# Zero fills spread over eight load steps instead of four, and row stores two steps later, in a kernel of attention and two expert layers

## What is computed

```python
# attention: B, H, S, D = 4, 8, 768, 48
for t in range(S):
    kt, vt, rt = (k[:, :, t], v[:, :, t], r[:, :, t])
    cur = np.einsum('bhd,bhe->bhde', u[None] * kt, vt)
    y[:, :, t] = np.einsum('bhd,bhde->bhe', rt, state + cur)
    state = w[None, :, :, None] * state + np.einsum('bhd,bhe->bhde', kt, vt)

# experts: N, D, E, F = 3072, 384, 8, 1024
e_idx = np.argmax(x @ w_gate, axis=1)
for e in range(E):
    mask = e_idx == e
    h = np.maximum(x[mask] @ w1[e], 0.0)
    out[mask] = gate_w[mask, None] * eom[mask, e, None] * (h @ w2[e])

# feed-forward: 3072 x 384, width 1536
g = x @ w_gate
val = x @ w_val
out = (silu(g) * val) @ w_out
```

## Time and profile before

| what | us |
|---|---|
| median of 3 runs (932.32 to 932.51) | 932.42 |
| the profiled execution, whole | 924.97 |
| its span, first to last instruction | 922.8 |
| PE busy in the span | 852.6 (92%) |
| DVE busy | 362.8 (39%) |
| POOL busy | 276.7 (30%) |
| ACT busy | 249.6 (27%) |
| attention stage, start to the first load of sorted rows | 184.2 |

### The profile page before, as it was taken

One profiled execution on the slowest core, in us unless ns is written; L12 is line 12 of the kernel. 1 busy time (PEld: TensorE's weight loads), 2 busy tenths in 40 slices (PEclk: granted clock), 3 DMA queues, 4 the chain that ended last, 5 costly groups with the idle time before them and its releaser, 6 DMA issues.

```text
span 922.8 us, 15994 instructions
## 1 busy us (share of the span) xinstructions
PE 852.6 (92%) x6056; PEld 771.7 (84%) x6056; DVE 362.8 (39%) x646; ACT 249.6 (27%) x457; POOL 276.7 (30%) x209
## 2 busy tenths in 40 slices
PE   7788898969889889889999999999999999999996
PEld 6677797869789789789978888888888888888885
DVE  7777979733442542542122222222222231232221
ACT  1212221113432432434343321222222122122211
POOL 5567857403443443544534110010001001001001
PEclk9987989979999999999999999999999999999999
DMA  9896645253443443344512000000000000000000
GB/s 187 220 225 147 141 104 116 82 127 92 114 121 101 117 118 101 116 114 119 154 52 52 1 35 0 1 21 14 0 0 34 0 0 34 0 0 34 1 1 35
DMA packets 138888, 67.66 MB, mean 73 GB/s; under 512 B 86232, under 2 KB 136536, under 8 KB 138840
## 3 DMA queue, kind: packets, MB, share of 16 engines
q1 hardware_dynamic: 135768, 57.34, 25.3%
q0 software_dynamic: 3072, 9.65, 2.7%
HBM read 51.97 MB, written 15.00 MB: 73 GB/s over the span
## 4 chain that ended last, share of the span: by engine, by line
PE 60%; issue 13%; POOL 7%; DVE 5%; DMA 2%; ACT 0%; POOLq 0%; SPq 0%; DVEq 0%; ACTq 0%
PE bank L1127 18%; PE bank L1129 18%; PE bank L1128 18%; POOL w_lo L513 7%; DMA xg<-x_sorted 1%; PE bank L1081 1%; PE bank L1102 1%; DVE xs L815 1%; PE bank L1071 1%; DVE attn L636 1%; PE bank L1135 0%; DVE x_out L661 0%; PE bank L1007 0%; PE bank L1039 0%; DMA token_at<-xg 0%
## 5 line engine op out<-in xcount | busy, mean ns | idle before, releaser
L513 POOL TENSOR_TENSOR w_lo<-raw,w_hi 128x768 fp32r<-128x768 f32 x64 | 117.4, 1838 | 156.5 <-ACT w_hi L902 155.7
L870 DVE TENSOR_TENSOR act<-silu,bank 128x512 f32<-128x512 f32 x72 | 49.5, 688 | 287.3 <-PE bank L1129 276.7
L565 POOL DMA_INDIRECT out_dram<-o_out,sorted_token x24 | 23.5, 980 | 380.1 <-ACT o_out L986 374.6
L1128 PE MATMUL bank<-bT,f_hi_late 128*128 (+1 forms) x288 | 112.8, 392 | 0.0
L1129 PE MATMUL bank<-bT,f_lo_late 128*128 (+1 forms) x288 | 112.8, 392 | 0.0
L1127 PE MATMUL bank<-bT,f_hi_late 128*128 (+1 forms) x288 | 112.1, 389 | 0.0
L1127 PE MATMUL bank<-h_hi,w_hi 128*128 128x416 f32 x192 | 73.2, 381 | 21.6 <-ACT y_all L940 21.6
L978 ACT ACTIVATE silu<-bank 128x512 f32<-128x512 f32 x72 | 43.1, 598 | 175.5 <-PE bank L1129 175.5
L980 ACT CAST act_hi<-act 128x512 fp32r<-128x512 f32 x72 | 44.7, 621 | 157.4 <-DVE act L870 157.4
L825 DVE SCALAR_TENSOR_TENSOR h_lo<-bank,h_hi 128x416 fp32r<-128x416 f32 x64 | 37.8, 591 | 100.5 <-ACT h_hi L934 100.5
L1128 PE MATMUL bank<-h_lo,w_hi 128*128 128x416 f32 x192 | 70.7, 368 | 0.0
(11 more groups left out here) (164 smaller groups left out, 1667.7 us busy)
## 6 DMA issues: line engine op xcount, KB each, us to landing
raw<-in_moe_w_dram SPq DMA_DIRECT2D x128, 192.0 KB, 2.5
x_sorted<-zeros SPq DMA_DIRECT2D x8, 651.6 KB
xg<-x_sorted SPq DMA_DIRECT2D x8, 651.6 KB
k_in<-in_k_dram SPq DMA_DIRECT2D x24, 192.0 KB, 3.3
r_in<-in_r_dram SPq DMA_DIRECT2D x24, 192.0 KB, 3.9
v_in<-in_v_dram SPq DMA_DIRECT2D x24, 192.0 KB, 4.1
raw<-in_moe_w_gate_dram SPq DMA_DIRECT2D x12, 192.0 KB, 2.5
raw<-in_moe_w_val_dram SPq DMA_DIRECT2D x12, 192.0 KB, 2.7
```

Of the source, the lines that this page charges most:

```text
L513: pool.tensor_tensor(w_lo[:, f, :], raw[:, f % RAW, 0:WC], w_hi[:, f, :].bitcast(F32), ALU.subtract).then_inc(w_split, 1)
L565: pool.indirect_dma_start(out[:, :], bass.IndirectOffsetOnAxis(sorted_token[:, m * BT + t:m * BT + t + 1].bitcast(U32), 0), o_out[:, t, :] ...
L870: dve.tensor_tensor(act[:, par, :], silu[:, par, :], bank[1][:], ALU.mult).then_inc(act_made, 1)
L1128: pe.matmul(ps, a_hi, b_lo_, start=False, stop=False)
```

## The change

The eight fills no longer go out two behind each of the four loads of chunk 1, but one behind each of the eight loads of chunks 1 and 2; in chunk 2 they stand between the load and the weight chunk. The wait for all fills moves from behind GpSimd's step 7 to behind its step 9. Each store moves two steps later: store i - 10 follows step i, and 13 to 23 follow step 23. The diff:

```diff
-                STORE_AFTER.setdefault(min(i + 2 * B, STEPS - 1), []).append(i)
+                STORE_AFTER.setdefault(min(i + 2 * B + 2, STEPS - 1), []).append(i)
...
                     load_qkv(c, b)
-                    if c == 1:
-                        for e in range(E // B * b, E // B * (b + 1)):
-                            fill(e)
+                    if c in (1, 2):
+                        fill(B * (c - 1) + b)
                     if c == 2:
                         sp.wait_ge(w_split, b + 1)
                         load_chunk(0, RAW + b)
...
                 attention_step(i)
-                if i == 2 * B - 1:
+                if i == 2 * B + 1:
                     pool.wait_ge(filled, 16 * E)
                 for n in STORE_AFTER.get(i, ()):
                     store_rows(n)
```

## The result

The change made the kernel slower by 0.47%: 935.14 us against 931.07 us, medians of 20 executions each on one chip, ratio 1.0047 with a 95% interval of 1.0027 to 1.0068. The forecast was 929.6 us with a range up to 934.3 against a before of 932.42; the sign is wrong, and the ratio lies above what the upper end of the range meant (934.3 / 932.42 = 1.0020).

A forecast was written before the change was run, and what follows sets the result against it. Transfers were taken to set the pace from 20 to 62 us. Later x_made(9) +0.6, step 10's clock -2.57 and stores -0.82 gave -2.8 us, from 932.42 to 929.6 us; range 926.5 to 934.3.

The forecast's parts named there:

- Which bound takes over: At GpSimd's k_pad(10), the wait for all fills takes back the whole 9 us gained by earlier loads.
- The landing of fill 7: In SyncE's queue, the last fill lands at 73.3 us, bounds 69.6 and 75.4.
- my list: Transfer rates tried for the last fill's landing: 221, 231 and 251 GB/s.
- second way: Last fill's landing from load 8 at 61.40 us plus three loads with chunks at 251 GB/s, 11.8 us: 73.2.
- the two ways: Last fill's landing by bytes at 231 GB/s, 73.3 us, and from load 8's landing, 73.2 us.
- The wait one for one: From k_pad(10) to x_made(9) the distance stays, so x_made(9) comes 0.6 us later; bounds 3.1 earlier, 2.7 later.
- The gain of 1.65 us: In step 9, should VectorE's L654 start ahead of k_pad(11), the step would end 1.65 us earlier.
- TensorE at the wait by 65 us: In the attention stage, TensorE was to be at step 9 by 65 us.
- The clock in step 10: TensorE runs step 10 at full clock after an idle of 1.7 to 3.2 us: 2.57 us gained.
- The stores: GpSimd's slot wait behind step 12 goes, 0.82 us gained; two more stores behind step 23 cost nothing.
- rival (C): Fill 7 lands at 75.4 us or later, the queue keeping 221 GB/s; +1.9 us, 934.3 us; chance 0.13.
- The transfers' share of 0.87: Over the early stretch the 16 transfer engines were busy only to 0.87, counted as room against rival (C).

The follow-up runs named there:

- e11: The changed kernel, unchanged, profiled a second time in one execution; the whole execution took 930.94 us.
- e2: The changed kernel with the wait for the fills behind step 11 instead of 9 and stores two more steps later; 921.61 us, ratio 0.9974 to before.
- e1: The kernel before with only the stores moved two steps later, fills and wait kept; 924.06 us, ratio 1.0003 to before.
- e12: The kernel before, unchanged, profiled a second time in one execution; the whole execution took 925.73 us.
- e5: The changed kernel with each fill issued ahead of its load instead of behind it; 930.15 us, ratio 1.0004 to before.
- e3: The changed kernel with each fill written from 32 partitions of 13 rows instead of 104 of 4; 927.33 us, ratio 1.0047 to before.
- e7: e2 plus ten spare TensorE products ahead of the wait for x_made in steps 6, 10 and 14; 917.86 us, ratio 0.9878 to before.
- e8: The kernel before plus ten spare TensorE products ahead of the wait for x_made in steps 6, 10 and 14; 923.23 us, ratio 0.9939 to before.
- e6: The changed kernel plus ten spare TensorE products ahead of the wait for x_made in steps 6, 10 and 14; 927.37 us, ratio 0.9997 to before.

## Why the prediction was wrong, point by point

**Which bound takes over.** Right. The wait for the fills, moved to k_pad(10), takes back all that the earlier loads give, and the row says so in the form that was forecast: 9.38 us (12.79 in e11; forecast 9 to 13), ended by x_sorted<-zeros. e2 shows it from the other side.

**The landing of fill 7: the term that failed.** I put it at 73.3 us with bounds of 69.6 and 75.4; k_pad(10) started at 76.58 and 76.73. Of the 6.9 us between the forecast of -2.8 and the +4.1 that came, 3.5 are this term (+0.6 forecast, +4.1 measured), 2.57 the clock and 0.82 the stores. The bytes were right, 10.64 MB. From 27.2 to 76.5 us they moved at 216 GB/s, which is below the slowest rate of my list. My second way had priced loads and chunks at 251 GB/s, from the stretch of 62 to 79 us, which holds no fills; and that set the load at 2.35 us and the fill at 3.3. The changed kernel allows a cleaner reading. One load and one fill take 6.03 us (31.85 to 37.88, 6.04 to 43.92) and one load and two fills took 9.0. So a fill is 2.97 us and a load 3.06. With the chunk, a cycle of three is 7.4 us (50.39 to 72.69 in three), which leaves 1.40 for the chunk. Then 27.2 + 8 x 2.97 + 7 x 3.06 + 3 x 1.40 = 76.6. That this meets the trace to 0.1 us is in part luck: the prices come from the same profile, its first pair took only 4.65 us (27.20 to 31.85), and with the cycle of e1 (8.39 us instead of 9.0) the load would come out at 3.7 us and the fill at 2.4. The same transfer, a load, took 2.35 us by the drain's rate and 3.06 in a mixed queue. That is 7 x 0.7 = 5 us over the stretch, less 8 x 0.33 by which I had the fill too dear. Nor did the prediction add up its own prices: 27.24 + 8 x 3.3 + 7 x 2.35 + 3 x 1.57 is 74.8, not 73.3. Its second way came out lower because it started from the measured 61.40, and of the four cycles before that the first had taken 7.14 us only (27.24 to 34.38). That I took the middle "because the two ways meet there" was no evidence: the 231 GB/s of the one and the 251 of the other are both from stretches behind the last fill.

**The wait one for one.** Right in kind: behind k_pad(10) the distance to x_made(9) stayed as it was (10.05 us in both profiles of the changed kernel and in the first of before), so in the first pair the 4.10 us arrive there whole; in e12 it was 10.89 us, with 1.16 us of waiting for a load ahead of k_pad(11). From k_pad(10) to the first load of a window it took 111.1 to 112.8 us in eight of the ten profiles without spare products; the others are after (118.9, with its stall) and e5 (108.9, with the clock back early). VectorE's decay lies beside k_pad(11) again, which started first (80.94 us against 81.05), and took 2.29 us against 2.21. The gain of 1.65 us that the prediction held open did not come, and e5 shows that it would not have come with the order reversed either. That TensorE would restart at half clock was right (transposes 1.12 us), though behind an idle of 4.54 us and not of 9.

**TensorE at the wait by 65 us.** Wrong, without effect. Step 6 waited 4.06 us for x_made and ran at half clock, and TensorE was through with step 9's product at 73.1 us. I had not looked at that step, though it is the same pattern as step 10. e3 and e11, where the engines came to the wait earlier, have the same landing; only the length of the wait differs.

**The clock in step 10.** Wrong: 2.57 us were counted as gained, and the product took 2.02 us after an idle of 2.90. I had put the idle at 1.7 to 3.2 us and taken the good end. In e11 the same product took 1.13 us after 3.41 us of idle, and the clock fell behind it (state product 0.88). That may be why in that pair only 2.3 of the 4.0 us were left at k_pad(12). So this term differs between executions of one kernel and should have been carried as a range. In both profiles the half clock also reached into step 11, which the prediction did not have at all: state times r took 1.89 and 1.77 us there and 1.13 in before and e12, and k_pad(13), which waits for step 11's state product, lost another 1.1 us (the table's steps from +4.10 to +5.22 and from +2.28 to +3.37).

**The stores.** The 0.82 us at step 12 were not gained: the slot wait is gone, and k_pad(13) waits longer in its place, 2.09 us. It starts in the same instant, 101.40 us, as VectorE's first instruction behind step 11's state product. By the code both wait for `state_mm` of step 11, so behind the slot wait stood a wait for TensorE. e1 has the same without the fills: 7.22 us from k_pad(12) to k_pad(13), before 7.24. That two more stores at the end cost nothing was right as far as e1 shows.

**The sum by what was measured.** At k_pad(13), first pair: +4.1 for the landing, 0 for the clock in step 10, +1.1 for the half clock in step 11, 0 for the stores, +5.2 us. Second pair: +4.0, then -0.8 by x_made(9), -0.9 in step 10, +1.1 in step 11, +3.4 us. Between the medians are 4.1 us; that the landing alone gives the same figure is luck. It is rival (C), with its mechanism as written (a fill in every stretch keeps the queue at its slow pace), without the 0.82 us at the stores that (C) counted as gained too, and with a landing 1.2 us beyond its threshold: the landing at 75.4 was its beginning, and its price grows one for one behind it. I gave it 0.13 and let the range end where it began. The transfers' share of 0.87, which I read as room, was none: after has 0.92 at the same rate.

## What to carry to other kernels

Price a transfer by a stretch in which the queue holds the same mixture as it will after the change; the pace of a stretch without the slow kind is no centre. Here that was the 221 GB/s of 20 to 62 us, which gave 75.4 us and was still 1.2 us short. Two mixtures can be solved for the price of each kind, but e3 shows that such prices need not hold in a third. When transfers are spread to relieve what waits for each of them, look for who waits for the last one: the same bytes must pass before it, and spreading pays only if that waiter moves behind the landing as well (here two steps more: e2, and resolved in e7 against e8). A short wait that disappears is a gain only if the next condition of the same instruction was met earlier, and this must be read from the code, since the profile names one releaser only.

## What was not expected of the hardware

- **A fill's price by its form.** The same 0.667 MB, in the old order and with a load at 3.06 us: 2.97 us from 104 partitions, 1.96 us from 128 (with 32 rows apart), 3.6 us from 32. The four executions of the first form differ among themselves by 0.4 us a fill (cycles of 8.39 to 9.19 us). Spread one by one between loads, the form from 32 partitions cost hardly more than that from 104 (landing at 77.08 against 76.58 us).
- **The clock and the idle ahead.** State times r took 2.02 us (1.2 GHz) behind idles of 2.90, 3.48 and 4.06 us, but 1.13 us behind 3.41 in e11, 3.36 in e3 and 3.13 in e1. Behind an idle of 2.72 us in step 14 it took 2.02 us in before and 1.13 us in after, and this goes with the kernel: of the ten profiles without spare products, all with 2.71 or 2.72 us of idle there, the four that wait for the fills at step 10 (after, e3, e5, e11) have 1.13 us and the six others 2.02. The length of the idle does not decide alone; what does is open. With the idle filled by spare products, state times r took 1.13 us in step 10 of e6 and the clock was at 1.00 in e7's steps 6 and 10; the kernel before gains 0.6% by them.
- **The distance between two profiles of one kernel.** The two of after differ by 7.2 us at the end of the attention stage and by 4.0 us in the whole. The first pair of profiles alone would have made the effect more than twice as large as it is.
